# A feed-forward product that takes its two column pieces in turn, weight by weight

## The chip, the cores and the metric

The kernel runs on one core of a Trainium2 chip. The metric is the device time of one execution in microseconds (us), lower is better. Times of an unprofiled execution are medians; spans and durations inside the kernel come from one profiled execution. Engines are TensorE (PE; its weight loads stand apart as PEld), VectorE (DVE), ScalarE (ACT), GpSimd (POOL) and SyncE (SP, which here issues transfers).

## The reference

Three stages follow each other. The change lies in the second, in `np.maximum(un @ w_ch1, 0.0) @ w_ch2`.

```
# 1. attention: batch 2, 8 heads, 768 rows, 64 wide; keys masked by hash bucket
# 2. Fourier mixing and a feed-forward network, d_model 512, hidden 2048
X = np.fft.fft(np.fft.fft(x, axis=1), axis=2)
u = x + np.real(X)
un = (u - mean(u)) / np.sqrt(var(u) + 1e-06)
x = u + np.maximum(un @ w_ch1, 0.0) @ w_ch2
# 3. gate: a causal convolution of 5 taps, sigmoid, and two 512x512 products
out = (sigmoid(conv(x)) * (x @ w_val)) @ w_out
```

## The kernel before

The feed-forward part works on transposed data: `unT` holds the 512 features of `un` in 4 blocks of 128 partitions (`KB` = 4), with the 768 rows of a batch as columns. The hidden layer is cut into 16 blocks of 128 features (`FB` = 16). They are numbered through both batches: n = 0 to 15 is batch 0, n = 16 to 31 batch 1. Each product is made of three, with operands split into a high and a low part: weight high by data high, weight low by data high, weight high by data low.

A matmul takes at most 512 columns here, so the 768 columns are cut into two pieces, `CH = [(0, 512), (512, 256)]`. Piece 0 of the hidden block is summed in PSUM bank 6 and piece 1 in bank 7 (`h_bank`).

For each block n there are four steps.

- `ffn1(n)`, the first product (L1549): 24 matmuls, 4 feature blocks x 3 terms x 2 pieces. After each piece it raises `h_full`.
- `relu(n)` on ScalarE (L831): evicts each piece with a relu into `h_hi`.
- `relu_lo(n)` on VectorE (L1143): reads each piece again and writes what rounding left into `h_lo`, and raises `h_lo_done` once per piece. After this the piece's bank is free.
- `ffn2(n)`, the second product (L1563): 24 matmuls, 4 output blocks x 3 terms x 2 pieces, added into banks 0 to 5. It takes each weight for 512 columns and then for 256.

TensorE's order is written out by hand: `ffn1(n + 1)` stands before `ffn2(n)`, so the eviction of a block lies beside a second product. `ffn1(n)` waits for block n - 1's eviction, since both use banks 6 and 7. In blocks 0 to 5 of batch 0, `ffn2(n)` has four transposes in it, after its first output block (`transpose_un(6 + n)`, L1468). They write a tile of batch 1's `un` to bank 6 (`un_bank`), so they wait until VectorE has read piece 0 of the newest block, `h_lo_done` at 2(n + 1) + 1. ScalarE (`unT_hi`, L799) and VectorE (`unT_lo`, L1112) then take the tile out, and the next first product waits for that.

After `ffn2(15)` batch 0's result is taken out of banks 0 to 5 (`take_x2`), while TensorE does `ffn1(16)`. Then 24 transposes of X (L1535) open batch 1's sums, and `ffn1(17)` follows.

GpSimd makes the low parts of the weights (L563, L568) and SyncE loads them, two blocks ahead.

Of the kernel before, what the change touches and what calls it, by code (L numbers as in the profile page):

```python
# [6 lines left out]
def attention_fft_ffn_gate_kernel(nc, qT, kT, v, proj, w_ch1, w_ch2, w_val, conv_wT, w_out,  # L7
# [25 lines left out]
    T = S // P  # L33
# [4 lines left out]
    KB = DM // P  # L38
# [10 lines left out]
    CH = [(0, C0), (C0, C1)]  # L49

    ctx = ExitStack()
    with ctx:
        def sb(name, shape, dt=F32, where=ctx):
            return where.enter_context(nc.sbuf_tensor(name, shape, dt))

        def sem(name):
            return ctx.enter_context(nc.semaphore(name))
# [8 lines left out]
        w1_hi = sb("w1_hi", [P, 2, KB, P], F32R)  # L66
        w1_lo = sb("w1_lo", [P, 2, KB, P], F32R)
# [96 lines left out]
        un_hi = [un0_hi, un1_hi]  # L164
        un_lo = [un0_lo, un1_lo]
# [44 lines left out]
        unT_lo_done = sem("unT_lo_done")  # L210
# [6 lines left out]
        h_full, h_hi_done, h_lo_done = sem("h_full"), sem("h_hi_done"), sem("h_lo_done")  # L217
# [14 lines left out]
        def need(eng, semaphore, value):  # L232

            if not isinstance(value, int) or value > 0:
                eng.wait_ge(semaphore, value)
# [1056 lines left out]
        def _(pe):  # L1292
# [245 lines left out]
            def ffn1(n, b, slot):  # L1538


                need(pe, w1_lo_done, n + 1)
                for c, (at, size) in enumerate(CH):

                    need(pe, h_lo_done, n * 2 + (c - 1))
                    if c == 0 and isinstance(n, int) and 2 <= n <= T:
                        pe.wait_ge(unT_lo_done, T + n - 1)
                    for kb in range(KB):
                        for m, (w_, x_) in enumerate(((w1_hi, un_hi[b]), (w1_lo, un_hi[b]), (w1_hi, un_lo[b]))):
                            op = pe.matmul(h_bank[c], w_[:, slot, kb, :], x_[:, kb, at:at + size],  # L1549
                                           start=(kb == 0 and m == 0), stop=(kb == KB - 1 and m == 2))  # L1550
                    op.then_inc(h_full, 1)

            def ffn2(n, slot, last):

# [15 lines left out]
            pe.wait_ge(parts_ready, 2 * (4 + 3))  # L1570
            pe.wait_ge(unT_lo_done, T)
            ffn1(0, 0, 0)
            pe.wait_ge(sin_copied, 3 * B)
            pe.wait_ge(parts_ready, 8 * B)
# [3 lines left out]
            for n in range(1, T + 1):  # L1578
                ffn1(n, 0, n % 2)
                ffn2(n - 1, (n - 1) % 2, False)  # L1580
            pe.wait_ge(unT_lo_done, B * T)
            with pe.Fori(T // 2, FB // 2 - 1) as j:
                ffn1(2 * j + 1, 0, 1)
                ffn2(2 * j, 0, False)
                ffn1(2 * j + 2, 0, 0)
                ffn2(2 * j + 1, 1, False)
# [154 lines left out]
```

## Time and profile before

| what | value |
|---|---|
| time, median of 3 runs | 635.16 us (634.46 to 636.32) |
| the profiled execution's own time | 635.57 us |
| its span, first to last instruction | 633.9 us |
| granted TensorE clock, mean | 0.997 |
| TensorE busy | 618.7 us, 98% of the span |
| VectorE, ScalarE, GpSimd busy | 346.1, 317.4, 250.7 us |
| feed-forward part in the span | about 286 to 564 us |

A busy time of 98% says that TensorE seldom stood still, not that it ran at its peak: a matmul's recorded duration overlaps the next one's. What a matmul costs in a row of them is the distance from its start to the next one's start. Lines are those of the kernel before.

### The profile page before, as it was taken

Reading aid. Unit: us, or ns where it says so; the run is one execution under the profiler, and the core shown is the slowest. Engines: PE = TensorE matmul, PEld = TensorE weight load, DVE = VectorE, ACT = ScalarE, POOL = GpSimd, SP = SyncE. Lnnn points to the kernel's source line nnn. Section 1 sums busy time; section 2 is a strip of 40 time slices with the busy share of each in tenths; the row PEclk is TensorE's granted clock in tenths of the full one; section 3 lists DMA queues with packets and bytes.
Section 4 is the critical chain, followed back from the end, with each engine's and each line's share of the span. In section 5 each row is a group of like instructions: output and inputs, shape, how many; then the busy total and the mean of one; then the engine's idle time right before and its main releaser. Section 6 shows DMA issues by size and latency. Waiting matters only on the chain.

```text
span 633.9 us, 11055 instructions
## 1 busy us (share of the span) xinstructions
PE 618.7 (98%) x3766; PEld 505.4 (80%) x3766; DVE 346.1 (55%) x587; ACT 317.4 (50%) x609; POOL 250.7 (40%) x213
## 2 busy tenths in 40 slices
PE   5899999999999999989999999999999999999998
PEld 4676777767777676989888888888888888888786
DVE  2888888887888875787111111117333333349820
ACT  3777777777777883464333222225233332444242
POOL 4533444333347664346333233327444434403140
PEclk9999999999999999999999999999999999999999
DMA  5762323223333020000211222620222221000202
GB/s 133 193 151 71 88 63 88 73 76 87 80 103 90 12 64 1 1 1 23 79 48 53 66 66 66 199 68 13 87 66 66 66 66 49 1 1 2 83 18 99
DMA packets 34267, 42.15 MB, mean 66 GB/s; under 512 B 3520, under 2 KB 22208, under 8 KB 34240
## 3 DMA queue, kind: packets, MB, share of 16 engines
q1 hardware_dynamic: 32272, 37.38, 20.6%
q0 software_dynamic: 1728, 4.02, 2.6%
q10 hardware_dynamic: 240, 0.39, 0.3%
q8 instruction: 17, 0.28, 0.2%
q14 instruction: 10, 0.08, 0.0%
HBM read 38.63 MB, written 3.15 MB: 66 GB/s over the span
## 4 chain that ended last, share of the span: by engine, by line
PE 90%; DVE 4%; ACT 2%; issue 2%; POOL 1%; DMA 1%; ACTq 0%; POOLq 0%; DVEq 0%
PE banks L1563 21%; PE banks L1549 21%; PE banks L1346 12%; PE banks L1363 11%; PE banks L1413 10%; PE banks L1642 5%; PE banks L1386 2%; PE banks L1494 2%; PE banks L1626 2%; PE banks L1299 2%; DVE x_then_u_then_gate L1213 1%; DMA k_raw<-in_k 1%; PE banks L1421 1%; PE banks L1305 1%; PE banks L1468 1%
## 5 line engine op out<-in xcount | busy, mean ns | idle before, releaser
L1143 DVE SCALAR_TENSOR_TENSOR h_lo<-banks,h_hi 128x512 fp32r<-128x512 f32 x64 | 35.4, 558 | 169.4 <-ACT h_hi L831 169.4
L1012 DVE TENSOR_REDUCE row_min<-banks 128x1 f32<-128x768 f32 x96 | 91.7, 956 | 33.9 <-PE banks L1346 33.4
L718 ACT ACTIVATE prob<-banks,row_min 128x768 f32<-128x768 f32 x96 | 87.0, 906 | 31.3 <-DVE row_min L1012 31.2
L1549 PE MATMUL banks<-unT_hi,w_hi 128*128 128x512 f32 (+1 forms) x256 | 86.4, 338 | 0.2 <-DVE h_lo L1143 0.2
L1549 PE MATMUL banks<-unT_hi,w_lo 128*128 128x512 f32 (+1 forms) x256 | 86.3, 337 | 0.0
L1549 PE MATMUL banks<-unT_lo,w_hi 128*128 128x512 f32 (+1 forms) x256 | 86.2, 337 | 0.0
L1413 PE MATMUL banks<-ident,prob 128*128 128x128 f32 x576 | 79.3, 273 | 1.3 <-ACT probT L350 1.3
L563 POOL TENSOR_TENSOR w_lo<-w_stage,w_hi 128x512 fp32r<-128x512 f32 x32 | 45.3, 1414 | 86.6 <-ACT w_hi L749 86.6
L1413 PEld LDWEIGHTS banks<-ident,prob 128*128 128x128 f32 x576 | 68.1, 140 | 6.7 <-issue 1.8
L831 ACT ACTIVATE h_hi<-banks 128x512 fp32r<-128x512 f32 x64 | 31.2, 490 | 79.4 <-PE banks L1549 79.3
L1363 PE MATMUL banks<-probT,v_in 128*64 128x384 f32 x384 | 69.0, 494 | 0.0
L568 POOL TENSOR_TENSOR w_lo<-w_stage,w_hi 128x512 fp32r<-128x512 f32 x32 | 42.2, 1317 | 67.2 <-ACT w_hi L754 67.2
L1563 PE MATMUL banks<-h_lo,w_hi 128*128 128x512 f32 (+1 forms) x256 | 66.0, 339 | 0.0
L1563 PE MATMUL banks<-h_hi,w_hi 128*128 128x512 f32 (+1 forms) x256 | 66.0, 339 | 0.0
L1563 PE MATMUL banks<-h_hi,w_lo 128*128 128x512 f32 (+1 forms) x256 | 65.6, 338 | 0.0
L754 ACT CAST w_hi<-w_stage 128x512 fp32r<-128x512 f32 x32 | 19.9, 621 | 88.6 <-PE banks L1563 88.6
L1213 DVE SCALAR_TENSOR_TENSOR x_then_u_then_gate<-x2T,taps,x_then_u_then_gate 128x384 f32<-128x384 f32 (+1 forms) x64 | 58.9, 926 | 4.9 <-DVE x_then_u_then_gate L1213 2.6
L1346 PE MATMUL banks<-k_a,q_a 128*128 128x384 f32 x192 | 57.6, 381 | 3.8 <-POOL q_a L502 2.8
L350 ACT COPY probT<-banks 128x384 f32<-128x384 f32 x104 | 49.0, 479 | 22.4 <-PE banks L1413 22.1
L497 POOL TENSOR_TENSOR k_b<-k_raw,k_a 64x768 fp32r<-64x768 f32 x16 | 29.2, 1826 | 72.1 <-ACT k_a L701 72.0
L1346 PEld LDWEIGHTS banks<-k_a,q_a 128*128 128x128 f32 x192 | 30.0, 191 | 32.6 <-issue 29.7
L1549 PEld LDWEIGHTS banks<-unT_hi,w_hi 128*128 128x128 f32 x256 | 48.1, 188 | 7.3 <-DVE h_lo L1143 0.4
(156 smaller groups left out, 1191.0 us busy)
## 6 DMA issues: line engine op xcount, KB each, us to landing
w_stage<-in_moe_w_ch SPq DMA_DIRECT2D x64, 256.0 KB, 2.8
q_raw<-in_q SPq DMA_DIRECT2D x32, 192.0 KB, 3.3
k_raw<-in_k SPq DMA_DIRECT2D x30, 192.0 KB, 3.6
v_in<-in_v SPq DMA_DIRECT2D x16, 192.0 KB, 2.8
out<-y_out SPq DMA_DIRECT2D x12, 256.0 KB, 2.0
seq_tables_sb<-in_dft POOLq DMA_DIRECT2D x6, 386.0 KB, 3.5
wvo_stage<-in_moe_w_val SPq DMA_DIRECT2D x1, 1024.0 KB, 5.7
wvo_stage<-in_moe_w_out SPq DMA_DIRECT2D x1, 1024.0 KB, 8.9
```

Of the source, the lines that this page charges most:

```text
L350: copy(dst, src).then_inc(scratch_free[bank_of(i, use)], 1)
L563: pool.tensor_tensor(w1_lo[:, slot, :, :], w1_stage[:, slot, :, :], w1_hi[:, slot, :, :].bitcast(F32), ALU.subtract).then_inc(w1_lo_done, 1)
L568: pool.tensor_tensor(w2_lo[:, slot, :], w2_stage[:, slot, :], w2_hi[:, slot, :].bitcast(F32), ALU.subtract).then_inc(w2_lo_done, 1)
L718: act.activation(prob[s % 2][:, :, :], s_tile(s), ACT.Exp, bias=row_min[:, s:s + 1], scale=-1.0, accum_out=row_sum[:, s:s + 1]).then_inc(e ...
L1012: dve.tensor_reduce(row_min[:, s:s + 1], s_tile(s), AX.XY, ALU.min).then_inc(min_ready, 1)
L1143: dve.scalar_tensor_tensor(out=h_lo[:, slot, at:at + size], in0=h_bank[c], scalar=0.0, in1=h_hi[:, slot, at:at + size].bitcast(F32), op0=A ...
L1213: dve.scalar_tensor_tensor(out=dst, in0=src, scalar=weight, in1=dst, op0=ALU.mult, op1=ALU.add).then_inc(conv_step, 1)
L1346: op = pe.matmul(s_tile(s)[:, c, :], lhs[:, rows], rhs[:, c * HALF:(c + 1) * HALF], start=start, stop=not start)
L1363: op = pe.matmul(PS[g * D:(g + 1) * D, 7, 0:HALF], v_in[:, h, kt, :], probT[h][:, kt, g * HALF:(g + 1) * HALF], start=(kt == 0), stop=(kt ...
L1413: op = pe.transpose(bank[:, j * P:(j + 1) * P], prob[tile % 2][:, c, j * P:(j + 1) * P], ident[:, :])
L1549: op = pe.matmul(h_bank[c], w_[:, slot, kb, :], x_[:, kb, at:at + size], start=(kb == 0 and m == 0), stop=(kb == KB - 1 and m == 2))
L1563: op = pe.matmul(acc(d, c), w_[:, slot, cols], h_[:, slot, at:at + size], start=False, stop=last, skip_group_check=True)
```

## The change

`ffn1` no longer finishes piece 0 before it begins piece 1. Each of its 12 weight operands is used for the 512 columns and then at once for the 256. The wait for block n - 1's eviction, which was one per piece, becomes one at the start that asks for both pieces. `h_full` is still raised once per piece, at that piece's last matmul. No matmul is added or removed, and the other engines' instructions and their order stay the same.

```diff
                 need(pe, w1_lo_done, n + 1)
-                for c, (at, size) in enumerate(CH):
-
-                    need(pe, h_lo_done, n * 2 + (c - 1))
-                    if c == 0 and isinstance(n, int) and 2 <= n <= T:
-                        pe.wait_ge(unT_lo_done, T + n - 1)
-                    for kb in range(KB):
-                        for m, (w_, x_) in enumerate(((w1_hi, un_hi[b]), (w1_lo, un_hi[b]), (w1_hi, un_lo[b]))):
+                need(pe, h_lo_done, n * 2)
+                if isinstance(n, int) and 2 <= n <= T:
+                    pe.wait_ge(unT_lo_done, T + n - 1)
+                for kb in range(KB):
+                    for m, (w_, x_) in enumerate(((w1_hi, un_hi[b]), (w1_lo, un_hi[b]), (w1_hi, un_lo[b]))):
+                        for c, (at, size) in enumerate(CH):
                             op = pe.matmul(h_bank[c], w_[:, slot, kb, :], x_[:, kb, at:at + size],
                                            start=(kb == 0 and m == 0), stop=(kb == KB - 1 and m == 2))
-                    op.then_inc(h_full, 1)
+                            if kb == KB - 1 and m == 2:
+                                op.then_inc(h_full, 1)
```

On TensorE, in the middle of `ffn1(1)`, the kernel before has these rows, where the chain of 512 columns ends and that of 256 begins (`w1_hi`, `w1_lo` are the weight's parts, `unT0` is batch 0's data).

```order
L1549 MATMUL banks<-unT0_hi,w1_hi 128x512
L1549 MATMUL banks<-unT0_hi,w1_lo 128x512
L1549 MATMUL banks<-unT0_lo,w1_hi 128x512
L1549 MATMUL banks<-unT0_hi,w1_hi 128x256 [waits h_lo_done]
L1549 MATMUL banks<-unT0_hi,w1_lo 128x256
L1549 MATMUL banks<-unT0_lo,w1_hi 128x256
```

The wait in mid-chain is gone with the change, and the pieces alternate from the start of the product.

On TensorE, from the end of `ffn1(1)` to the transposes inside `ffn2(0)`, the kernel before has these rows.

```order
L1549 MATMUL banks<-unT0_hi,w1_hi 128x256
L1549 MATMUL banks<-unT0_hi,w1_lo 128x256
L1549 MATMUL banks<-unT0_lo,w1_hi 128x256
L1563 MATMUL banks<-h_hi,w2_hi 128x512 [waits w2_lo_done,h_lo_done]
L1563 MATMUL banks<-h_hi,w2_hi 128x256
L1563 MATMUL banks<-h_hi,w2_lo 128x512
L1563 MATMUL banks<-h_hi,w2_lo 128x256
L1563 MATMUL banks<-h_lo,w2_hi 128x512
L1563 MATMUL banks<-h_lo,w2_hi 128x256
L1468 MATMUL banks<-ident,un 128x128 [waits h_lo_done,un_ready]
```

At the same place on TensorE the changed kernel, whose first product stands on L1548, has these.

```order
L1548 MATMUL banks<-unT0_hi,w1_lo 128x512
L1548 MATMUL banks<-unT0_hi,w1_lo 128x256
L1548 MATMUL banks<-unT0_lo,w1_hi 128x512
L1548 MATMUL banks<-unT0_lo,w1_hi 128x256
L1563 MATMUL banks<-h_hi,w2_hi 128x512 [waits w2_lo_done,h_lo_done]
L1563 MATMUL banks<-h_hi,w2_hi 128x256
L1563 MATMUL banks<-h_hi,w2_lo 128x512
L1563 MATMUL banks<-h_hi,w2_lo 128x256
L1563 MATMUL banks<-h_lo,w2_hi 128x512
L1563 MATMUL banks<-h_lo,w2_hi 128x256
L1468 MATMUL banks<-ident,un 128x128 [waits h_lo_done,un_ready]
```

The last 512-column matmul stood 12 matmuls of 256 columns ahead of the second product; now only one stands between. The transposes and their wait are where they were.

## Rows read from the trace of the kernel before

**Rows 1.** The page: busy time (share) and instructions; the chain that ended last.

```profile
PE 618.7 (98%) x3766; PEld 505.4 (80%) x3766; DVE 346.1 (55%) x587; ACT 317.4 (50%) x609; POOL 250.7 (40%) x213
...
PE 90%; DVE 4%; ACT 2%; issue 2%; POOL 1%; DMA 1%; ACTq 0%; POOLq 0%; DVEq 0%
PE banks L1563 21%; PE banks L1549 21%; PE banks L1346 12%; PE banks L1363 11%; PE banks L1413 10%; PE banks L1642 5%; PE banks L1386 2%; PE banks L1494 2%; PE banks L1626 2%; PE banks L1299 2%; DVE x_then_u_then_gate L1213 1%; DMA k_raw<-in_k 1%; PE banks L1421 1%; PE banks L1305 1%; PE banks L1468 1%
```

**Rows 2.** Waits from 286 to 565 us: total, times, longest.

```profile
PEld banks L1549 <- DVE h_lo L1143: 0.4, 1, 0.4
...
PE banks L1549 <- DVE h_lo L1143: 0.2, 1, 0.2
```

**Rows 3.** Windows: length, busy us of PE, PEld, DVE, ACT, POOL, then PEclk.

```profile
286.24:345.00 58.76, 58.76 (x355) 52.02 (x354) 19.18 (x44) 22.27 (x40) 22.62 (x26) 1.00 0.19 54
...
442.00:555.00 113.00, 113.00 (x649) 99.12 (x648) 41.48 (x56) 38.62 (x69) 48.60 (x35) 1.00 0.20 58
```

**Rows 4.** Chain in batch 0's loop: start us, us, work, instructions.

```profile
346.45 4.21 PE banks L1549 x24
350.67 4.22 PE banks L1563 x24
```

**Rows 5.** The same chain in batch 1's loop.

```profile
450.56 4.18 PE banks L1549 x24
454.73 4.20 PE banks L1563 x24
```

**Rows 6.** TensorE, one first product: start us, us, engine, line, operation.

```profile
405.33 0.39 PE L1549 MATMUL banks<-unT_hi,w_hi 128*128 128x512 f32 x1
...
408.12 0.28 PE L1549 MATMUL banks<-unT_hi,w_hi 128*128 128x256 f32 x1
...
409.54 0.52 PE L1563 MATMUL banks<-h_hi,w_hi 128*128 128x512 f32 x2
```

**Rows 7.** The second product's weight loads and products: duration ns min/median/max.

```profile
L1563 PEld LDWEIGHTS banks<-h_hi,w_hi x256: 187/188/192, 297.2 to 562.5; 128*128 128x128 f32 x128
L1563 PE MATMUL banks<-h_hi,w_hi x256: 278/336/479, 297.3 to 562.7; 128*128 128x512 f32 x128
```

**Rows 8.** All engines around the transposes of turn 1.

```profile
304.49 0.39 PE L1549 MATMUL banks<-unT_lo,w_hi 128*128 128x512 f32 x1
...
304.92 0.60 ACT L831 ACTIVATE h_hi<-banks 128x512 fp32r<-128x512 f32 x1 [2.11 <-PE banks L1549]
...
305.56 0.69 DVE L1143 SCALAR_TENSOR_TENSOR h_lo<-banks,h_hi 128x512 fp32r<-128x512 f32 x1 [5.26 <-ACT h_hi L831]
...
306.14 0.52 PE L1563 MATMUL banks<-h_hi,w_hi 128*128 128x512 f32 x2
...
307.08 0.47 PEld L1468 LDWEIGHTS banks<-ident,un 128*128 128x128 f32 x4
307.20 0.60 PE L1468 MATMUL banks<-ident,un 128*128 128x128 f32 x4
...
308.46 0.69 DVE L1112 TENSOR_TENSOR unT_lo<-banks,unT_hi 128x512 fp32r<-128x512 f32 x1 [1.28 <-ACT unT_hi L799]
```

**Rows 9.** All engines around the transposes of turn 0.

```profile
296.07 0.60 ACT L831 ACTIVATE h_hi<-banks 128x512 fp32r<-128x512 f32 x1 [3.29 <-PE banks L1549]
...
296.77 0.69 DVE L1143 SCALAR_TENSOR_TENSOR h_lo<-banks,h_hi 128x512 fp32r<-128x512 f32 x1 [0.77 <-ACT h_hi L831]
...
297.30 0.52 PE L1563 MATMUL banks<-h_hi,w_hi 128*128 128x512 f32 x2
...
298.24 0.37 PEld L1468 LDWEIGHTS banks<-ident,un 128*128 128x128 f32 x3
```

**Rows 10.** All engines where batch 1 begins.

```profile
432.78 1.02 DVE L1143 SCALAR_TENSOR_TENSOR h_lo<-banks,h_hi 128x512 fp32r<-128x512 f32 x2 [3.97 <-ACT h_hi L831]
...
433.53 0.19 PEld L1549 LDWEIGHTS banks<-unT_hi,w_hi 128*128 128x128 f32 x1 [0.41 <-DVE h_lo L1143]
433.53 0.50 PE L1549 MATMUL banks<-unT_hi,w_hi 128*128 128x512 f32 x1 [0.18 <-DVE h_lo L1143]
```

## The prediction

> **What bounds the kernel now.** I read the page first. TensorE (PE) is busy 618.7 of 633.9 us, and 90% of the chain that ended last lies on it; the first product (L1549) and the second (L1563) hold 21% each [rows 1]. So whatever moves TensorE in the feed-forward part moves the end. The table of waits says what stops it there: from 286 to 565 us there is one wait of the first product, 0.2 us seen from its matmul and 0.4 us seen from its weight load, and no wait of the transposes [rows 2]. The windows confirm it: 58.76 of 58.76 us busy while batch 0 begins, 113.00 of 113.00 us in batch 1's loop, at a granted clock of 1.00, the 2.4 GHz level [rows 3]. VectorE and ScalarE are busy a third of that time or less. They are not the bound, but they decide when bank 6 comes free.
>
> **The pace of the two orders.** Both orders stand in the trace side by side, with the same work: 12 matmuls of 512 columns and 12 of 256. The first product has them chain by chain, the second in turn, as the change wants them for the first. The chain gives 4.21 us for the first and 4.22 for the second in batch 0 [rows 4], 4.18 and 4.20 in batch 1 [rows 5]. By single instructions, a 512-column matmul takes (408.12 - 405.33) / 12 = 0.2325 us and a 256-column one (409.54 - 408.12) / 12 = 0.118 us, together 0.351 us [rows 6]; a pair of the second product takes 4.22 / 12 = 0.352 us [rows 4]. So giving each weight to both pieces in turn saves nothing in the second product. Its rows also say why: 256 loads stand there for 256 matmuls [rows 7], so the weight is loaded again for the second piece, and the load (188 ns) runs under the matmul before it. I price the new order at the second product's pace: 16 blocks x 0.01 us + 16 x 0.02 us = 0.5 us more. Bounds: nothing, and 32 x 0.02 = 0.6 us.
> The Trainium skill, "TensorE: Matmul & The Clock Gate", section "Step-by-step: what each phase is for", says that separate loads let one load a weight once and use it repeatedly. By that rule the change might gain; in this trace the same weight for two pieces has two loads [rows 7]. If that rule held here, it would be the second rival below.
>
> **What the change moves: when the pieces are complete.** The 512-column piece was complete after 12 of 24 matmuls, 1.4 us before the first product ended, and its eviction (relu on ScalarE, the low part on VectorE) began while TensorE worked on the other piece. Now both end together. Nobody needs the low part in the loops soon: the next first product begins one second product (4.2 us) later. But three kinds of places are tighter.
>
> *The six transposes of batch 1 that ride in batch 0's second products.* For blocks 0 to 5, after a quarter of the second product, four transposes write bank 6, which is where the 512-column piece lies. They wait until VectorE has read it (h_lo_done). I work it out for block 1 [rows 8]. Before: the last 512-column matmul starts at 304.49, relu at 304.92 (0.43 later), VectorE at 305.56 (0.64 later), and ends at 305.56 + 0.69 = 306.25. The transposes' weight load starts at 307.08, so 0.83 us were to spare. Now the last 512-column matmul starts one pair before the second product: 306.14 - 0.35 = 305.79. Relu then starts at 306.22, VectorE at 306.86 and ends at 307.55. From such an end to the waiting weight load the trace has about 0.05 us (432.78 + 0.70 = 433.48, load at 433.53) [rows 10], so the release comes at 307.60. The load was due at 307.08: TensorE waits 0.52 us. The wait sits on the load and not on the matmul [rows 10], so nothing of it is hidden. Behind it queue the remaining three quarters of the second product and everything after, with no gap later that could take it up. Block 0 is the same with a slower handover: the load stands 298.24 - 297.30 = 0.94 us after the second product began, as in block 1 (307.08 - 306.14), and relu to VectorE is 0.70 us instead of 0.64 [rows 9], so it waits 0.58 us. Sum: 0.58 + 5 x 0.52 = 3.2 us. Bounds: if only the matmul waited and the load went ahead, 0.12 us less each, 2.5 us; if ScalarE took 0.1 us longer to begin because the second piece arrives together with the first, 3.8 us.
> What is late next: the transposed tiles. Their low part was begun at 308.46 and took 0.69 [rows 8], so ended at 309.15; first products last about 4.2 us and the next begins near 310.8. Everything shifts together by 0.5 us, so the 1.6 us to spare stay.
>
> *The first product after the transposes of X that open batch 1.* It used to wait for VectorE's first piece only; now it waits for both at its start. The two VectorE pieces run from 432.78 to 433.80, and the product started at 433.53 [rows 10]. With 0.05 us to the load, the start moves to 433.85: 0.3 us more. This wait is already on the path, so it counts in full. Bounds 0.2 and 0.4.
>
> *All other first products.* They too ask for both pieces at the start. With the eviction beginning at the end of the first product, by block 1's rows (0.43 + 0.64 + 0.69, then 0.4 for the small piece) both are read about 1.9 us after the last pair begins, and the next first product begins 4.2 us after. Cost nothing while that cover stands; if VectorE were 2.6 us late, it would cost what exceeds it. The wait in mid-chain goes away; it showed no idle time, so it gives nothing.
>
> **Sum.** 3.2 + 0.3 + 0.5 = 4.0 us on the profiled execution's 635.57, so 639.6. That execution stands 0.4 us above the median of the three runs, 635.16; on the median the sum gives 639.1 us.
>
> **Rivals.**
> *Half of it comes back.* If the second load of a weight already in place cost less, some of the 4.0 us would return. Splitting 0.2325 and 0.118 us into a part per column and a part per matmul gives (2 x 0.118 - 0.2325) = 4 ns per matmul; saved once per pair, 384 x 4 ns = 1.5 us, so 637.6. With waits at their low bound it would be about 636.8, not to be told from no change, which for this kernel is anything within 0.3% (1.9 us). Against it: the second product already has this order and is not faster. Some 0.1 for an outcome within 0.3%.
> *Faster: loads were what set the pace.* At 2.4 GHz, 512 columns alone would take 213 ns and 256 columns 107, so 19 + 11 = 30 ns per pair are not columns. If all of that were load time and repeating a weight took it away, 384 x 30 ns = 11.5 us would go and the time be 635.2 + 3.5 - 11.5 = 627. It decides from 14 ns per pair on ((3.5 + 1.9) / 384). For it: the weight engine is busy 99 of 113 us [rows 3]. Against: the second product's pace again. 0.04.
> *Slower by more: the eviction is slower when it runs under the second product.* ScalarE then evicts two pieces in a row, and the release comes later. With 0.5 us more in each of six places the time is 639.1 + 3.0 = 642. For it: the ready pieces now arrive together; against: the first piece is first in both queues. 0.08.
>
> **How the numbers follow.** The forecast as summed has 0.78, the slower rival 0.08, the two others 0.10 and 0.04. Slower by over 0.3%: 0.86; within: 0.10; faster: 0.04. The terms' bounds give 2.5 + 0.2 + 0 = 2.7 and 3.8 + 0.4 + 0.6 = 4.8 us, 637.9 to 640.0; medians of three of this kernel spread by about 1 us either way, and the range takes in part of both neighbours: 637.2 to 641.2.
>
> **What would show it.** In the profile after: six waits of the transposes' weight load on VectorE's low part, some 0.5 us each, where there were none; relu starting about 0.1 us after the second product does; the first product's 24 instructions at 4.20 to 4.22 us; the wait at the start of batch 1 0.3 us longer. The prediction is wrong if the pair in the first product takes clearly under 0.351 us, or if the transposes don't wait.

## The result, and the profile after

The changed kernel takes 639.38 us (median of 5 runs, 638.81 to 639.70), the kernel before in the same comparison 634.46 us. The ratio is 1.0072, with a 95% interval of 1.0056 to 1.0089. It is slower by 4.6 us, by that ratio. The span of the profiled execution grew from 633.9 to 637.7 us.

The time of one kernel goes with the mean granted clock of the execution: in the comparison of the first four experiments below, the kernel before took 633.78 us at 1.00, 634.86 at 0.997 and 636.90 at 0.992 (medians of 6, 19 and 4 executions). The feed-forward part itself runs at 1.00 in every profile, so its length shows differences of about 1 us better than the times do.

The page of the changed kernel looks almost like that of before [rows 1]: 2.2 us more of busy TensorE, one percentage point less of its share.

```profile
PE 620.9 (97%) x3766; PEld 506.1 (79%) x3766; DVE 345.9 (54%) x587; ACT 314.0 (49%) x609; POOL 246.8 (39%) x213
...
PE 89%; DVE 4%; ACT 3%; issue 2%; POOL 1%; DMA 1%; SPq 0%; ACTq 0%; DVEq 0%; POOLq 0%
PE banks L1548 21%; PE banks L1563 20%; PE banks L1346 12%; PE banks L1363 10%; PE banks L1413 10%; PE banks L1642 5%; PE banks L1386 2%; PE banks L1494 2%; PE banks L1626 2%; PE banks L1299 2%; DVE x_then_u_then_gate L1213 1%; PE banks L1468 1%; PE banks L1421 1%; DMA q_raw<-in_q 1%; PE banks L1305 1%
```

The table of waits, from 286 to 570 us, is where the change shows. Columns: total us, times, longest.

```profile
PEld banks L1468 <- issue: 3.8, 6, 0.7
...
PE banks L1468 <- DVE h_lo L1143: 2.1, 6, 0.4
...
PEld banks L1548 <- DVE h_lo L1143: 0.7, 1, 0.7
PE banks L1548 <- DVE h_lo L1143: 0.5, 1, 0.5
```

Before, no transposes (L1468) stood in it and the first product's load waited once, 0.4 us [rows 2]. Now six groups of four transposes wait, and the load at the start of batch 1 waits 0.7 us. The first row is a lesson in reading: the load's wait is put down to "issue", that is to nothing that the profile shows, yet the matmul that belongs to it names the releaser, VectorE's `h_lo`. The 3.8 us also hold the 0.05 us or so for which the weight engine idles before any pair's load.

One such place, block 1, in all engines' order of time. It answers to [rows 8].

```profile
305.70 0.52 PE L1548 MATMUL banks<-unT_lo,w_hi 128*128 128x512 f32 x2
...
306.05 0.51 PE L1563 MATMUL banks<-h_hi,w_hi 128*128 128x512 f32 x2
306.13 0.87 ACT L831 ACTIVATE h_hi<-banks 128x512 fp32r<-128x512 f32 x2 [3.42 <-PE banks L1548]
...
306.76 1.02 DVE L1143 SCALAR_TENSOR_TENSOR h_lo<-banks,h_hi 128x512 fp32r<-128x512 f32 x2 [6.58 <-ACT h_hi L831]
307.57 0.42 PEld L1468 LDWEIGHTS banks<-ident,un 128*128 128x128 f32 x4 [0.63 <-issue]
307.60 0.63 PE L1468 MATMUL banks<-ident,un 128*128 128x128 f32 x4 [0.34 <-DVE h_lo L1143]
```

The last 512-column matmul starts at 305.70, one pair before the second product. ScalarE follows at 306.13, VectorE at 306.76, and the weight load of the transposes, due at 306.05 + 0.94 = 306.99, starts at 307.57. ScalarE now evicts both pieces one right behind the other (x2 is two instructions).

The chain that ended last makes the same detour. Columns: start us, us, work, instructions.

```profile
302.00 4.11 PE banks L1548 x23
...
306.13 0.61 ACT h_hi L831
...
306.76 0.70 DVE h_lo L1143
...
307.60 0.63 PE banks L1468 x4
308.23 3.15 PE banks L1563 x18
311.38 4.11 PE banks L1548 x23
```

Before, the chain stayed on TensorE all through this stretch. Now it leaves it for ScalarE and VectorE six times. A turn, from first product to first product, takes 311.38 - 302.00 = 9.38 us.

In batch 1's loop the chain stays on TensorE, but the first product takes 4.24 us where it took 4.18 [rows 5].

```profile
449.21 4.21 PE banks L1563 x24
453.42 4.24 PE banks L1548 x24
```

Windows of the two corresponding stretches (length, busy us of PE, PEld, DVE, ACT, POOL, PEclk): TensorE stands still 2.1 us where batch 0 begins, and nowhere in batch 1's loop. The granted clock is 1.00 as before [rows 3], the 2.4 GHz level. The 2.1 us is less than what the waits cost: in block 1 the matmul before the transposes is recorded to 306.75 + 0.51 = 307.26, but the next one would have started at about 307.11 (0.36 us after it, as before), so part of the delay counts as busy.

```profile
286.24:348.00 61.76, 59.69 (x354) 51.67 (x353) 17.97 (x43) 20.83 (x40) 22.41 (x25) 1.00 0.17 51
...
446.00:555.00 109.00, 109.00 (x621) 95.29 (x620) 41.30 (x55) 32.55 (x65) 40.96 (x32) 1.00 0.20 59
```

Where batch 1 begins, the load now follows the end of VectorE's second piece (435.19 + 1.02 = 436.21), not of its first [rows 10].

```profile
435.19 1.02 DVE L1143 SCALAR_TENSOR_TENSOR h_lo<-banks,h_hi 128x512 fp32r<-128x512 f32 x2 [3.97 <-ACT h_hi L831]
...
436.26 0.30 PEld L1548 LDWEIGHTS banks<-unT_hi,w_hi 128*128 128x128 f32 x2 [0.73 <-DVE h_lo L1143]
```

Added up from the chains, the feed-forward part (first start of the first product to the last end of the second) went from 563.73 - 286.40 = 277.3 us to 567.55 - 285.71 = 281.8 us: 3.15 us up to the first product of block 7 (60.05 us after the start before, 63.20 after), 0.3 us at the start of batch 1, 1.0 us in batch 1's loop and the rest in the product between. The part before it was 0.7 us shorter in this one execution, which is why the spans differ by 3.8 and not by 4.5.

### The profile page after: what moved, and what is told of

Read it like the earlier page. It is cut to its first block, busy times and chain, and to the rows that moved or that the text cites. A ratio compares the mean times of both kernels' runs of the same rounds, so it can differ in the third digit from the quotient of the medians.

```text
span 637.7 us, 11055 instructions
## 1 busy us (share of the span) xinstructions
PE 620.9 (97%) x3766; PEld 506.1 (79%) x3766; DVE 345.9 (54%) x587; ACT 314.0 (49%) x609; POOL 246.8 (39%) x213
## 3 DMA queue, kind: packets, MB, share of 16 engines
HBM read 38.63 MB, written 3.15 MB: 66 GB/s over the span
## 4 chain that ended last, share of the span: by engine, by line
PE 89%; DVE 4%; ACT 3%; issue 2%; POOL 1%; DMA 1%; SPq 0%; ACTq 0%; DVEq 0%; POOLq 0%
PE banks L1548 21%; PE banks L1563 20%; PE banks L1346 12%; PE banks L1363 10%; PE banks L1413 10%; PE banks L1642 5%; PE banks L1386 2%; PE banks L1494 2%; PE banks L1626 2%; PE banks L1299 2%; DVE x_then_u_then_gate L1213 1%; PE banks L1468 1%; PE banks L1421 1%; DMA q_raw<-in_q 1%; PE banks L1305 1%
## 5 line engine op out<-in xcount | busy, mean ns | idle before, releaser
L1143 DVE SCALAR_TENSOR_TENSOR h_lo<-banks,h_hi 128x512 fp32r<-128x512 f32 x64 | 32.7, 553 | 175.7 <-ACT h_hi L831 175.7
L563 POOL TENSOR_TENSOR w_lo<-w_stage,w_hi 128x512 fp32r<-128x512 f32 x32 | 41.9, 1310 | 99.7 <-ACT w_hi L749 99.7
L831 ACT ACTIVATE h_hi<-banks 128x512 fp32r<-128x512 f32 x64 | 27.9, 488 | 95.4 <-PE banks L1548 95.4
L1548 PE MATMUL banks<-unT_lo,w_hi 128*128 128x512 f32 (+1 forms) x256 | 66.2, 340 | 0.0
L1548 PE MATMUL banks<-unT_hi,w_lo 128*128 128x512 f32 (+1 forms) x256 | 66.1, 340 | 0.0
L1548 PE MATMUL banks<-unT_hi,w_hi 128*128 128x512 f32 (+1 forms) x256 | 65.6, 337 | 0.5 <-DVE h_lo L1143 0.5
L568 POOL TENSOR_TENSOR w_lo<-w_stage,w_hi 128x512 fp32r<-128x512 f32 x32 | 41.7, 1304 | 62.3 <-ACT w_hi L754 62.2
L1213 DVE SCALAR_TENSOR_TENSOR x_then_u_then_gate<-x2T,taps,x_then_u_then_gate 128x384 f32<-128x384 f32 (+1 forms) x64 | 61.5, 966 | 4.9 <-DVE x_then_u_then_gate L1213 2.6
L350 DVE COPY probT<-banks 128x384 f32<-128x384 f32 x88 | 48.3, 548 | 3.1 <-PE banks L1413 3.1
```

The source lines that it names most:

```text
L350: copy(dst, src).then_inc(scratch_free[bank_of(i, use)], 1)
L563: pool.tensor_tensor(w1_lo[:, slot, :, :], w1_stage[:, slot, :, :], w1_hi[:, slot, :, :].bitcast(F32), ALU.subtract).then_inc(w1_lo_done, 1)
L568: pool.tensor_tensor(w2_lo[:, slot, :], w2_stage[:, slot, :], w2_hi[:, slot, :].bitcast(F32), ALU.subtract).then_inc(w2_lo_done, 1)
L1143: dve.scalar_tensor_tensor(out=h_lo[:, slot, at:at + size], in0=h_bank[c], scalar=0.0, in1=h_hi[:, slot, at:at + size].bitcast(F32), op0=A ...
L1213: dve.scalar_tensor_tensor(out=dst, in0=src, scalar=weight, in1=dst, op0=ALU.mult, op1=ALU.add).then_inc(conv_step, 1)
```

## The experiments

Ratios are to the kernel before, run on the same chip in the same comparison. A "turn" is one first and one second product. The length of the feed-forward part, read from the chain of each profile as above (from the start of block 0's first product to the end of block 31's second), tells the kernels apart: profiles that should be alike agree within 0.02 us (281.84, 281.82 and 281.83; 277.46 twice).

| kernel | feed-forward part, us | over the kernel before |
|---|---|---|
| before | 277.3 | |
| changed | 281.8 | +4.5 |
| changed, transposes a quarter later | 278.7 | +1.4 |
| changed, last feature block in chains | 279.6 | +2.2 |
| changed, last two in chains (two profiles) | 277.5 | +0.1 |
| before, one wait at the start | 277.7 | +0.3 |
| new order in batch 0 alone | 280.8 | +3.4 |
| new order in batch 1 alone | 278.7 | +1.4 |
| changed, no weight repeated | 281.8 | +4.5 |
| before, second product in chains | 277.6 | +0.2 |
| changed, tiles shifted by 64 bytes | 282.5 | +5.2 |
| changed, tiles shifted by 512 bytes | 281.8 | +4.5 |
| last two in chains, eviction ahead of the tap | 276.9 | -0.5 |

**Transposes a quarter later.** In the changed kernel:

```diff
-                    if d == 1 and isinstance(n, int) and n < T:
+                    if d == 2 and isinstance(n, int) and n < T:
                         transpose_un(T + n)
```

> The changed kernel, with the four transposes of each of the blocks 0 to 5 one quarter of the second product later (after its second output block instead of its first). Theory (the transposes wait for bank 6, about 0.5 us in six places): they come due 1.05 us later, when VectorE has long read piece 0, so the waits go away and each of these turns is 8.85 us instead of 9.38; the time falls by 3.1 us against the changed kernel, to a ratio of about 1.002 to the kernel before. Rival (the new order itself is slower in batch 0, by whatever cause): the turns stay at 9.3 to 9.4 us and the ratio near 1.007.

Measured: 636.52 us, ratio 1.0022 (1.0009 to 1.0035). The chain of a turn in batch 0:

```profile
301.76 4.21 PE banks L1548 x24
305.98 2.11 PE banks L1563 x12
308.08 0.44 PE banks L1468 x4
308.52 2.11 PE banks L1563 x12
```

The transposes come after 12 instructions of the second product, and nothing waits: the next first product starts 8.87 us after this one. The new order of the first product is untouched here, so it was the wait for bank 6, and not the order by itself, that lengthened these turns. What is left, 1.4 us of the feed-forward part, is batch 1's: the 0.3 us at its start and its slower first product (4.24 us).

**Last feature block in chains, and last two.** In the changed kernel the order of the 24 matmuls became (k is 1 or 2):

```diff
+                order = [(kb, m, c) for kb in range(KB - k) for m in range(3) for c in range(2)]
+                order += [(kb, m, c) for c in range(2) for kb in range(KB - k, KB) for m in range(3)]
...
```

> The changed kernel, but for the last of the four feature blocks the first product does its three 512-column matmuls and then its three of 256. Piece 0 is complete 0.24 us earlier. Theory of the bank wait: a wait of 0.5 us becomes one of 0.28 (six of them 1.7 instead of 3.2 us), turns of 9.13 us in batch 0's first blocks; time 1.4 us under the changed kernel. Rival (the handover between products costs a fixed amount however early piece 0 is complete): turns stay at 9.38.

Measured: 637.51 us, ratio 1.0045 (1.0031 to 1.0059).

```profile
304.01 4.21 PE banks L1551 x24
308.23 1.05 PE banks L1566 x6
309.27 0.10 issue
309.37 0.63 PE banks L1468 x4
...
313.16 4.21 PE banks L1551 x24
```

A turn is 313.16 - 304.01 = 9.15 us, as the theory of the bank wait has it (9.13), and not 9.38. So a piece that is complete 0.24 us earlier gives back 0.23 us. The feed-forward part fell by 2.3 us against the changed kernel, not by the 1.4 expected, since batch 1's first product also came back, from 4.24 to 4.20 us. That was not foreseen.

> The changed kernel, but the last two feature blocks go in chains: six 512-column matmuls, then six of 256. Piece 0 is complete 0.59 us earlier than in the changed kernel. Theory of the bank wait: the release comes when the transposes are due or just before, so six waits of zero to 0.06 us, turns of 8.86 to 8.9 us; time 3.1 us under the changed kernel. Rival of the fixed cost: 9.38 still. The start of batch 1 keeps its longer wait (0.3 us).

Measured: 634.29 us, ratio 0.9992 (0.9981 to 1.0004); in a second comparison 635.24 us, 1.0004 (0.9989 to 1.0019). Turns in batch 0 and in batch 1:

```profile
301.81 4.21 PE banks L1551 x24
306.02 1.05 PE banks L1566 x6
307.07 0.44 PE banks L1468 x4
307.51 3.16 PE banks L1566 x18
```

```profile
450.33 4.17 PE banks L1551 x24
454.51 4.21 PE banks L1566 x24
```

No wait of the transposes, turns of 8.86 us. The feed-forward part fell by 4.4 us against the changed kernel, not by the 3.1 expected, since batch 1's first product also went from 4.24 to 4.17 us. That was not foreseen either. Batch 1's load still waits 0.7 us at its start.

**The one wait at the start, alone.** In the kernel before:

```diff
+                need(pe, h_lo_done, n * 2)
                 for c, (at, size) in enumerate(CH):
 
-                    need(pe, h_lo_done, n * 2 + (c - 1))
```

> The kernel before with its chains as they were, only the wait for both pieces of the eviction moved to the start of the first product. Theory: nothing changes in the loops, and the first product that opens batch 1 starts 0.3 us later; ratio 1.0005, within noise. Rival (the one wait at the start is what costs, in many places): first products start late throughout and the ratio is over 1.002.

Measured: 634.54 us, ratio 0.9994 (0.9981 to 1.0007). The time can't tell 0.3 us from nothing; the table of waits can, and so can the feed-forward part, which is 0.3 us longer.

```profile
PEld banks L1549 <- DVE h_lo L1143: 0.7, 1, 0.7
PE banks L1549 <- DVE h_lo L1143: 0.5, 1, 0.5
```

The load's wait at the start of batch 1 is 0.7 us instead of 0.4 [rows 2], the same as in the changed kernel. Nothing else waits for `h_lo`. So this small term is the merged wait's, and nothing but this term is.

**New order in one batch alone.** In the changed kernel, with the condition `b == 0` in one and `b == 1` in the other (the one wait at the start stays in both):

```diff
+                if b == 0:
+                    order = [(kb, m, c) for kb in range(KB) for m in range(3) for c in range(2)]
+                else:
+                    order = [(kb, m, c) for c in range(2) for kb in range(KB) for m in range(3)]
...
```

> The changed kernel, but the first product alternates its pieces in batch 0 alone; in batch 1 it has its chains back (the one wait at the start stays everywhere). Theory: the six waits of the transposes (0.52 to 0.58 us each) stay, the 0.3 us at the start of batch 1 stays, batch 1's first product falls from 4.24 back to 4.18 us. Sum 3.2 + 0.3 = 3.5 us over the kernel before, ratio 1.0055, and 1 us under the changed kernel.

> The changed kernel, but the first product alternates its pieces in batch 1 alone. Theory: no wait of the transposes, turns of 8.86 us in batch 0's first blocks; batch 1's first product 4.24 us instead of 4.18 and the longer wait at its start: 0.9 + 0.3 = 1.2 us over the kernel before, ratio 1.002. Rival (a wait in batch 0 that has nothing to do with the new order): ratio 1.005 or more.

Measured: batch 0 alone 637.49 us, ratio 1.0051 (1.0033 to 1.0069); batch 1 alone 636.57 us, ratio 1.0032 (1.0016 to 1.0049). In the first, the six waits stand as in the changed kernel and batch 1's first product is back at 4.18 us. In the second, no transposes wait and it is at 4.24. The feed-forward part is 3.4 us longer in the first and 1.4 in the second; the 0.3 us at the start of batch 1 is in both, so together they make up the whole 4.5. By its time the second came out above the 1.002 expected, which its interval still holds; its feed-forward part is near the 1.2 us expected.

**Same alternation, no weight repeated.** In the changed kernel piece 1 runs one weight ahead:

```diff
+                for i in range(3 * KB):
+                    for c, (at, size) in enumerate(CH):
+                        kb, m = divmod((i + c) % (3 * KB), 3)
...
```

> The changed kernel, but piece 1 runs one weight ahead of piece 0: 512 and 256 columns still alternate, yet no two neighbouring matmuls have the same weight. Same matmuls and loads. Theory (each matmul's load is there anyway, so a repeated weight is worth nothing): 4.21 us per first product in batch 0 and 4.24 in batch 1, turns of 9.38 us, as in the changed kernel. Rival (repeating a weight saves something that alternation costs elsewhere): first products slower, 4 ns per pair or more, 4.26 us in batch 0.

Measured: 638.75 us, ratio 1.0069 (1.0046 to 1.0092). Batch 1's loop:

```profile
452.11 4.24 PE banks L1551 x24
456.35 4.21 PE banks L1566 x24
```

4.24 and 4.21 us, as in the changed kernel, and 4.21 for both in batch 0; the feed-forward part is the same too. That two neighbours share their weight is worth nothing here. This settles the two rivals that needed a cheaper repeated load.

**The second product in chains.** In the kernel before:

```diff
-                    for w_, h_ in ((w2_hi, h_hi), (w2_lo, h_hi), (w2_hi, h_lo)):
-                        for c, (at, size) in enumerate(CH):
+                    for c, (at, size) in enumerate(CH):
+                        for w_, h_ in ((w2_hi, h_hi), (w2_lo, h_hi), (w2_hi, h_lo)):
```

> The kernel before with the opposite change in the second product: for each output block three matmuls of 512 columns, then three of 256, where it took them in turn. Nothing waits differently. Theory (alternating costs a few ns per pair in batch 1 and nothing in batch 0): second product 4.21 us in batch 0 and 4.18 in batch 1 instead of 4.20; ratio 0.999 to 1.000. Rival (batch 1's slower pace belongs to the first product alone, by its operands): second product stays at 4.20.

Measured: 635.49 us, ratio 1.0013 (0.9996 to 1.0029).

```profile
449.94 4.17 PE banks L1549 x24
454.12 4.22 PE banks L1563 x24
```

The theory fails, and so does the rival, which had the second product stay at 4.20: in batch 1 it got slower by 0.02 us, and a turn takes 8.39 us against 8.38 (8.44 against 8.43 in batch 0). The first product, which is untouched and whose operands lie where they did, moved by about as much (4.17 from 4.18, and 4.24 from 4.21 in batch 0). So single products of a turn shouldn't be read to the last hundredth, and the order in the neighbouring product is one of the things that move them. So chains are not the faster order as such. What the few nanoseconds per pair come from, this run does not show.

**Tiles shifted by 64 and by 512 bytes.** In the changed kernel (16 or 128 elements):

```diff
+        pad = sb("pad", [P, 16])
         un1_hi = sb("unT1_hi", [P, KB, S], F32R)
```

> The changed kernel with an unused tile of 64 bytes per partition ahead of the batch 1 data of the first product, so that its operands, and all tiles behind them, lie 64 bytes further from the weights. Nothing else. Open is why the alternating first product takes 4.21 us in batch 0 and 4.24 in batch 1. Theory (where the operands lie against each other sets it): some of the four paces, 4.21, 4.21, 4.24 and 4.21, move by 0.02 us or more. Rival (what runs on the other engines in batch 1 sets it): they stay as they are. Waits as in the changed kernel either way.

> The same with 512 bytes. Theory and rival as for the shift by 64 bytes.

Measured, one execution each: 640.39 us with 64 bytes, 641.89 us with 512. The latter had a mean clock of 0.992, with 0.94 up to 60 us and 0.96 from 240 to 285 us, both ahead of the part that matters, so its time is not compared. The paces with 64 bytes, batch 0 and then batch 1:

```profile
358.00 4.24 PE banks L1549 x24
362.24 4.24 PE banks L1564 x24
```

```profile
458.73 4.23 PE banks L1564 x24
462.96 4.21 PE banks L1549 x24
```

The first product now takes 4.24 us in batch 0 and 4.21 in batch 1, the reverse of the changed kernel, and the second 4.24 and 4.23 instead of 4.21. By whole turns batch 0 lost 0.05 us (8.48 from 8.43) and batch 1 gained 0.01 (8.44 from 8.45), and the feed-forward part grew by 0.7 us. With 512 bytes everything is back at 4.21 and 4.21 us in batch 0, 4.24 and 4.21 in batch 1.

So where the operands lie moves the pace by up to 0.03 us per product, 2 or 3 ns per pair of matmuls. The old order with shifted tiles was not run.

**ScalarE's eviction ahead of the convolution tap.** On top of the last two blocks in chains:

```diff
+            relu(FB, 0)
             with act.Fori(0, FB // 2 - 1) as j:
                 first_tap(0, j)
                 for u in range(2):
-                    relu(FB + 2 * j + u, u)
+                    if u:
+                        relu(FB + 2 * j + u, u)
...
                 act.copy(wvo_hi[:, j, :], wvo_stage[:, j, :]).then_inc(wvo_hi_done, 1)
+                relu(FB + 2 * j + 2, 0)
             first_tap(0, 2 * KB - 1)
-            relu(2 * FB - 2, 0)
...
```

> The kernel with the last two feature blocks in chains, and in batch 1 ScalarE evicts each even block before it begins the next convolution tap (0.7 us) instead of after. Theory: at the start of batch 1 both pieces are read 0.7 us earlier, at about the time that the transposes of X end, so the wait of 0.7 us of the first product's weight load falls to 0.0 to 0.1; time 0.7 us under the kernel with the last two blocks in chains alone, ratio 0.998 to the kernel before. Rival (VectorE's convolution taps, now begun 0.7 us later, delay a later eviction): the wait comes back at the next first product and the ratio stays at 0.999.

> The kernel with the last two feature blocks in chains once more, beside the one with the earlier relu on the same chip. Theory: ratio 0.999, turns of 8.86 us.

Measured: 633.79 us, ratio 0.9994 (0.9983 to 1.0006), beside 635.24 for the same kernel without it. The chain where batch 1 begins:

```profile
428.32 2.62 PE banks L1537 x24
430.94 4.36 PE banks L1553 x24
```

It stays on TensorE from the transposes of X (L1537 here) into the first product; the wait of 0.7 us is gone and none came in its place. The feed-forward part is 0.6 us shorter than without the earlier eviction, near the 0.7 expected. Of the 1.45 us between the two medians a part is the mix of granted clocks: among the executions at 0.997 the medians are 634.65 (7) and 635.32 us (8), 0.7 apart. The interval against the kernel before holds 1, so by its time the kernel can't be called faster than that one; its feed-forward part is 0.5 us shorter.

## Why the prediction was right

**The main term, six waits for bank 6: right in place and size.** Predicted 3.2 us, measured 3.15 us in the chain. The steps held one by one in block 1: relu 0.08 us after the second product began (predicted 0.08), VectorE 0.63 later (0.64), its first piece 0.70 (0.69). Two small errors cancelled. The load followed VectorE's end by 0.11 us and not 0.05, so it waited 0.58 us, not 0.52. But its first matmul stands 0.03 us behind it instead of 0.12, and the second product went on 0.39 us after that matmul instead of 0.36, so the turn grew by 0.52. That it is the wait, and that it goes as the time at which the piece is complete, is shown: 0.52 us, 0.29 and nothing for the piece complete 0, 0.24 and 0.59 us earlier, and nothing with the transposes a quarter later.

**The start of batch 1: right.** Predicted 0.3 us, measured 0.3, and the merged wait alone brings it.

**The pace of the new order: too small, and for a reason that doesn't hold.** Predicted 0.5 us in all, 0.01 us per block in batch 0 and 0.02 in batch 1, with 0.6 us as the upper bound. Measured: nothing in batch 0 (a turn of 8.43 us both before and after) and 1.0 us in batch 1 (8.38 to 8.45 us, 14 turns). The step that failed is the pricing by the second product's pace, as if alternating had a price of its own. It has none that is the same everywhere: the second product in chains is no faster, the first product in whole chains is no faster than with its first half alternating (4.18 and 4.17 us in batch 1), and 64 bytes of shift move both products' paces by as much. Nor does the loss in batch 1 spread evenly over the 12 pairs: with the last three of them in chains it is down from 0.06 to 0.02 us. That the placement of the operands moves the pace is shown, and that the order does at one and the same placement. That this kernel's placement happened to suit the old order in batch 1 is a guess; which operands matter, and by what mechanism, stays open.

**All other waits: right.** Both pieces' eviction after the end of the first product is covered in the loops, as nothing else waits for `h_lo`. Two readings on the way were off. By the prediction's own terms both pieces are read 0.43 + 0.64 + 0.69 + 0.4 = 2.2 us after the last pair begins, not 1.9; in block 1 of the changed kernel it is 306.76 + 1.02 - 305.70 = 2.1. And VectorE and ScalarE were busy 33 to 38% of the two stretches [rows 3], a little more than a third. Neither changes the sum.

**The rivals.** The cheaper repeated load, in its half and in its full form, is excluded by the kernel in which no weight repeats. The slower eviction didn't come: ScalarE took 0.87 us for both pieces.

The sum was 4.0 us, the chains show 4.5 and the ratio 4.6; the difference is the pace in batch 1. That the time itself, 639.38 us, lies so close to the predicted 639.1 is in part luck: the kernel before took 634.46 us in the comparison where the prediction had started from 635.16, and that lower start made up for the sum that was too small.

## What to carry to other kernels

Interleaving two accumulation chains makes both finish last. Ask who waits for the first one: not only its consumer, but whoever wants its bank next. Let the chain that is waited for first end early; here six matmuls of the other at the end were enough to take away all six waits. And look whether a shared weight saves a load in the trace before giving up an order for it.

## What the runs showed of the hardware that was not expected

A first product of 24 matmuls took 4.21 us in one batch and 4.24 in the other, with the same instructions. A shift of the tiles by 64 bytes swapped them, and slowed the second product from 4.21 to 4.24 and 4.23 us (one execution); a shift by 512 bytes changed nothing. The 64 bytes made the feed-forward part 0.7 us longer, 282.5 from 281.8 us, as much as some changes bring.
